# Half-array products of both chunks in one step, waits on GpSimd, more warming products and a new order in a WKV and Fourier-mixing kernel

## The reference

```
for t in range(S):                       # state is 48 x 48 per head
    cur = outer(u * k_t, v_t)
    y_t = r_t @ (state + cur)
    state = w_t[:, None] * state + outer(k_t, v_t)
x = heads side by side                   # 4 x 768 x 384
mixed = real(fft(fft(x, axis=1), axis=2))
u = x + mixed
un = (u - mean(u)) / sqrt(var(u) + 1e-6) # over the last axis
out = u + relu(un @ w_ch1) @ w_ch2
```

## Time and profile before

| | |
|---|---|
| three runs, us | 194.07, 197.35, 198.51 (median 197.35) |
| the profiled execution, us | 195.99, of which its span 194.2 |
| PE, DVE, ACT, POOL busy | 95%, 82%, 64%, 56% |
| HBM read and written | 23.59 MB, 4.72 MB |

### The profile page before, as it was taken

One profiled execution on the slowest core, in us unless ns is written; L12 is line 12 of the kernel. 1 busy time (PEld: TensorE's weight loads), 2 busy tenths in 40 slices (PEclk: granted clock), 3 DMA queues, 4 the chain that ended last, 5 costly groups with the idle time before them and its releaser, 6 DMA issues.

```text
span 194.2 us, 4751 instructions
## 1 busy us (share of the span) xinstructions
PE 184.4 (95%) x1830; PEld 118.5 (61%) x1830; DVE 159.9 (82%) x369; ACT 125.0 (64%) x293; POOL 108.1 (56%) x126
## 2 busy tenths in 40 slices
PE   7997899999997999979999999999899999999994
PEld 3565567577665666656666666765365676656663
DVE  7799985756999798999999999998998889574044
ACT  5799858347997669979778888962682251435200
POOL 2083993646968488486999499446957431000000
PEclk9999969969999999999999999999999999999999
DMA  5998989898998059999859798998475020521133
GB/s 140 312 290 201 217 168 211 152 196 171 177 187 150 0 119 212 204 208 219 185 112 225 124 218 179 192 215 148 91 160 135 0 84 6 130 66 44 41 122 122
DMA packets 107175, 29.79 MB, mean 153 GB/s; under 512 B 102033, under 2 KB 106770, under 8 KB 107154
## 3 DMA queue, kind: packets, MB, share of 16 engines
q1 hardware_dynamic: 105202, 27.14, 64.7%
q0 software_dynamic: 1952, 2.36, 7.5%
HBM read 23.59 MB, written 4.72 MB: 146 GB/s over the span
## 4 chain that ended last, share of the span: by engine, by line
PE 56%; DVE 21%; DMA 11%; issue 3%; ACT 3%; SPq 2%; POOL 2%; DVEq 0%; POOLq 0%
PE bank L1167 16%; PE bank L1149 15%; DMA w<-in_moe_w_ch_dram 6%; PE bank L1188 3%; PE bank L1101 3%; PE bank L1078 3%; DVE ah L817 3%; DMA unt<-un 3%; DMA in_r<-in_r_dram 2%; DVE ah L975 2%; PE bank L1018 2%; DVE x L868 2%; DVE uf L1103 1%; DVE bst L1107 1%; DVE rkh L517 1%
## 5 line engine op out<-in xcount | busy, mean ns | idle before, releaser
L1167 PE MATMUL bank<-w,ht 128*128 128x384 bf16 (+2 forms) x300 | 53.4, 320 | 1.3 <-DMA w<-in_moe_w_ch_dram 1.3
L1149 PE MATMUL bank<-unt,w 128*128 128x384 bf16 x288 | 53.3, 326 | 1.3 <-DVE uf L1103 0.6
L1156 ACT ACTIVATE ht<-bank 128x384 bf16<-128x384 f32 x73 | 33.7, 493 | 20.0 <-PE bank L1149 20.0
L1167 PEld LDWEIGHTS bank<-w,ht 128*128 128x128 bf16 x300 | 27.8, 98 | 17.0 <-DVE ah L817 1.4
L1149 PEld LDWEIGHTS bank<-unt,w 128*128 128x128 bf16 x288 | 26.3, 97 | 18.9 <-DVE uf L1103 1.0
L517 POOL TENSOR_TENSOR rk<-rk,ub 128x384 f32<-128x384 f32 x22 | 22.3, 1019 | 8.7 <-DVE rk L517 4.6
L817 DVE TENSOR_TENSOR ah<-bank,msk 128x512 bf16<-128x512 f32 x36 | 23.3, 678 | 0.9 <-PE bank L812 0.8
L517 POOL TENSOR_TENSOR rkh<-in_k,e 128x384 bf16<-128x384 f32 x14 | 15.7, 1127 | 11.4 <-DMA in_k<-in_k_dram 4.1
L1171 DVE SCALAR_TENSOR_TENSOR osb<-bank,rstd,uf 128x384 f32<-128x384 f32 (+2 forms) x25 | 14.8, 594 | 7.7 <-PE bank L1167 7.6
L517 POOL TENSOR_TENSOR vtd<-in_v,dc 128x384 f32<-128x384 f32 (+1 forms) x21 | 17.4, 830 | 5.5 <-DVE dc L924 3.2
L517 POOL TENSOR_TENSOR rk<-in_r,in_k 128x384 f32<-128x384 f32 x17 | 17.6, 1039 | 1.8 <-issue 1.8
(11 more groups left out here) (167 smaller groups left out, 380.6 us busy)
## 6 DMA issues: line engine op xcount, KB each, us to landing
out_dram<-osb SPq DMA_DIRECT2D x23, 192.0 KB, 2.2
in_v<-in_v_dram SPq DMA_DIRECT2D x18, 192.0 KB, 4.0
in_w<-in_w_dram SPq DMA_DIRECT2D x18, 192.0 KB, 4.1
in_k<-in_k_dram SPq DMA_DIRECT2D x18, 192.0 KB, 4.4
in_r<-in_r_dram SPq DMA_DIRECT2D x18, 192.0 KB, 4.0
w<-in_moe_w_ch_dram POOLq DMA_DIRECT2D x2, 1152.0 KB, 11.0
in_r<-in_r_dram SPq DMA_DIRECT2D x3, 384.0 KB, 5.2
in_w<-in_w_dram SPq DMA_DIRECT2D x3, 384.0 KB, 5.1
```

The costliest lines, as they stand in the source:

```text
L1149: ins = e.matmul(ps(t)[:, 0:384], W1[:, m, 128 * j:128 * j + 128], unt[:, :, m, :], start=(m == 0), stop=(m == NM - 1))
L1156: "act": lambda e, j=j, t=t, ht=ht: e.activation(ht[:, j, :], ps(t)[:, 0:384], ACTF.Relu, scale=-1.0)},
L1167: ins = e.matmul(ps(t)[:, 0:hi - lo], ht[:, j, 128 * x:128 * x + 128], W2[:, j, lo:hi], start=(j == 0), stop=(j == NJ - 1))
```

## The change

1. `tot`, `state` and `ymat` of a pair are each one step for both chunks: the products of chunk 0 (rows 0 to 63) and chunk 1 (rows 64 to 127) alternate, into different PSUM banks. The last pair has no totals and no state for its second chunk.
2. The state-carrying products leave these steps: `inter` (4 full-array products of 96 columns) and the identity product are steps of their own, after the half-array ones. Each of the five chunks after the first has one `inter`, four have an identity product.
3. A POOL step marked `port` waits for the DVE step marked `port` that the plan started last before it (`AHEAD`).
4. Warming products 8 -> 16.
5. Planned durations are changed, and `ORDER` is new for all engines. Counted by step, 124 steps change their engine: 34 from POOL to DVE, 26 from DVE to POOL, 30 from DVE to ACT, 28 from ACT to DVE, 4 from POOL to ACT, 2 from ACT to POOL. POOL has 112 steps instead of 122, 110 of them marked `port`.

Places in the new order that are spoken of below: of batch 0's `xf` folds, six go from POOL to DVE and two from DVE to POOL; its first two `hcr` steps go from POOL to ACT; chunk 5's copy of x from DVE to ACT. W2's DMA has 35 POOL steps ahead of it instead of 39, and the step just ahead but one is now `rkh` of batch 1's chunk 2, whose decay totals stand at PE place 107 (before: 62). On SP the first store of a result stands 43rd (before: 41st), and the load of v for batch 1's chunk 5 stands ahead of it (before: behind it); v of batch 0's last pair is the 21st issue instead of the 15th. Of the 16 warming products, one stands before the first decay sums, four among the first two pairs, six between the second `ymat` and the first product of the mix, five among the first L1101.

```diff
-DMA_T, DMA_U, T_RK, T_UN, T_XFER, T_PAIR, T_SC, T_Y = 15, 2, 1750, 2000, 1800, 1400, 450, 850
+DMA_T, DMA_U, T_RK, T_UN, T_XFER, T_PAIR = 15, 2, 1750, 2000, 1800, 1210
+T_SC, T_Y, T_ST, T_TOT = 250, 1050, 450, 450
...
-NW = 8
+NW = 16
...
+                    if self.AHEAD and e == "pool" and ahead is not None:
+                        s = max(s, ahead.end + self.LAT[e])
...
             if o.port:
                 port[e] = s + o.dur
+                if self.AHEAD and e == "pool" and ahead is not None:
+                    o.deps.add(ahead)
...
+            if o.port and e == "dve":
+                ahead = o
...
-        return int(50 + n * 2.36)
+        return int(50 + n * 2.45)
...
+        nl = 2 - (c0 + 2 == NC)
+        def tot(e):
+            for j in range(nl):
+                e.matmul(ps(tci[j])[:, DM:DM + H], IDB[:, :], NPB[:, :, :].rearrange("p h x -> p (h x)"), start=True,
+                         stop=False, skip_group_check=True)
+            for h in range(HP):
+                for i in range(2):
+                    for j in range(nl):
+                        x = e.matmul(ps(tci[j])[:, DM + 2 * h:DM + 2 * h + 2],
+                                     LB[i2[i]][64 * j:64 * j + 64, 2 * h:2 * h + 2, :].rearrange("t h d -> t (h d)"),
+                                     NON[64 * j:64 * j + 64, :], start=False, stop=(i == 1), skip_group_check=True)
+            return x
+        op("pe", T_TOT, tot, r=["NON", "IDB", "NPB"] + lb, w=tci[0:nl])
...
+        tds = [g.tile("a") for y in range(nl)]
+        def state(e):
+            for h in range(HP):
+                for i in range(2):
+                    for y in range(nl):
+                        x = e.matmul(ps(tds[y])[:, 96 * h:96 * h + 96],
...
+        op("pe", T_ST, state, r=[("KH", i) for i in i4] + vbs, w=tds, tiled=True)
+        ty = [g.tile("a") for y in range(2)]
+        def ymat(e):
+            for i in range(2):
+                for y in range(2):
+                    e.matmul(ps(ty[y])[:, 0:DM], PM[64 * y:64 * y + 64, 4 + i, :], vtb[i][64 * y:64 * y + 64, :],
+                             start=(i == 0), stop=False, skip_group_check=True)
+            for h in range(H):
+                for i in range(2):
+                    for y in range(2):
+                        x = e.matmul(ps(ty[y])[:, D * h:D * h + D], AH[i2[i]][64 * y:64 * y + 64, h, :],
...
+        op("pe", T_Y, ymat, r=ahs + vbs + [("PM", 4), ("PM", 5)] + [("VTD", m % 4) for m in ns], w=ty, tiled=True)
...
+            if c:
+                def inter(e, y=y, s_in=s_in):
+                    for q in range(HP):
+                        x = e.matmul(ps(ty[y])[:, 96 * q:96 * q + 96], RTB[i4[y]][:, q, :], s_in[:, q, :], start=False,
+                                     stop=True, skip_group_check=True)
+                    return x
+                op("pe", mm(96, 4), inter, r=rts + [("ST", (c + 1) % 2)], w=[ty[y]])
+            if y < nl:
+                if c:
+                    op("pe", mm(DM), lambda e, y=y, s_in=s_in: e.matmul(
+                        ps(tds[y])[:, 0:DM], IDB[:, :], s_in[:, :, :].rearrange("p h d -> p (h d)"), start=False, stop=True,
+                        skip_group_check=True), r=[("ST", (c + 1) % 2), "IDB"], w=[tds[y]])
```

More of the change, by code:

```diff
@@ L136 @@
     SWITCH = 95
+    AHEAD = 1
     def __init__(self, nc):
@@ L184, in schedule @@
         port = {"dve": 0, "pool": 0}
+        ahead = None
         bank = [None] * 8
@@ L771, in attention @@
            r=[("RK", i2)], w=[("DC", i2)])
-        op(None, {"pool": 787, "dve": v_1(DM)}, tt(vtd[:, :, :], vt[:, :, :],
+        op(None, {"pool": 820, "dve": v_1(DM)}, tt(vtd[:, :, :], vt[:, :, :],
                                                    dc[:, :].unsqueeze(2).to_broadcast([128, H, D]), ALU.mult),
@@ L898, in attention_pair @@
             op("act", a_ps(DM) + 20, lambda e, t=tce[j]: e.activation(ps(t)[:, 0:DM], ps(t)[:, 0:DM], ACTF.Exp), w=[tce[j]])
-        for j in range(2):
-            last = c0 + j == NC - 1
-            if not last:
-                def tot(e, j=j, t=tci[j]):
-                    e.matmul(ps(t)[:, DM:DM + H], IDB[:, :], NPB[:, :, :].rearrange("p h x -> p (h x)"), start=True,
-                             stop=False, skip_group_check=True)
-                    for h in range(HP):
-                        for i in range(2):
-                            x = e.matmul(ps(t)[:, DM + 2 * h:DM + 2 * h + 2],
-                                         LB[i2[i]][64 * j:64 * j + 64, 2 * h:2 * h + 2, :].rearrange("t h d -> t (h d)"),
-                                         NON[64 * j:64 * j + 64, :], start=False, stop=(i == 1), skip_group_check=True)
-                    return x
-                op("pe", mm(1, 9), tot, r=["NON", "IDB", "NPB"] + lb, w=[tci[j]])
-            ne = DM if last else DM + H
+        nl = 2 - (c0 + 2 == NC)
[11 more added lines that the diff above has]
+        op("pe", T_TOT, tot, r=["NON", "IDB", "NPB"] + lb, w=tci[0:nl])
+        for j in range(2):
+            ne = DM + H if j < nl else DM
             op("act", a_ps(ne), lambda e, j=j, ne=ne, t=tci[j]: e.activation(E2[i2[j]][:, 0:ne], ps(t)[:, 0:ne], ACTF.Exp,
@@ L926, in attention_pair @@
                r=[("RK", z)], w=[("DC", z)])
-            op(None, {"pool": 787, "dve": v_1(DM)}, tt(vtb[j].rearrange("p (h d) -> p h d", d=D), cut("v", j),
+            op(None, {"pool": 820, "dve": v_1(DM)}, tt(vtb[j].rearrange("p (h d) -> p h d", d=D), cut("v", j),
                                                        dc[:, :].unsqueeze(2).to_broadcast([128, H, D]), ALU.mult),
@@ L980, in attention_pair @@
         vbs = [("VB", n % 4) for n in ns]
+        tds = [g.tile("a") for y in range(nl)]
[4 more added lines that the diff above has]
+                        x = e.matmul(ps(tds[y])[:, 96 * h:96 * h + 96],
+                                     KH[i4[i]].rearrange("t h d -> t (h d)")[64 * y:64 * y + 64, 128 * h:128 * h + 128],
+                                     VB[ns[i] % 4][64 * y:64 * y + 64, 2 * h:2 * h + 2, :].rearrange("t h d -> t (h d)"),
+                                     start=(h == 0 and i == 0), stop=(i == 1), skip_group_check=True)
+            return x
@@ new lines, in attention_pair @@
+        op("pe", T_ST, state, r=[("KH", i) for i in i4] + vbs, w=tds, tiled=True)
[9 more added lines that the diff above has]
+                        x = e.matmul(ps(ty[y])[:, D * h:D * h + D], AH[i2[i]][64 * y:64 * y + 64, h, :],
+                                     VB[ns[i] % 4][64 * y:64 * y + 64, h, :], start=False, stop=(i == 1),
+                                     skip_group_check=True)
+            return x
@@ L981, in attention_pair @@
+        op("pe", T_Y, ymat, r=ahs + vbs + [("PM", 4), ("PM", 5)] + [("VTD", m % 4) for m in ns], w=ty, tiled=True)
         for y in range(2):
-            c, n = c0 + y, ns[y]
-            p0, p1 = 64 * y, 64 * y + 64
+            c = c0 + y
             s_in, s_out = ST[(c + 1) % 2], ST[c % 2]
-            ty = g.tile("a")
-            if c < NC - 1:
-                tds = g.tile("a")
-                def state(e, c=c, p0=p0, p1=p1, s_in=s_in, tds=tds):
-                    if c:
-                        e.matmul(ps(tds)[:, 0:DM], IDB[:, :], s_in[:, :, :].rearrange("p h d -> p (h d)"),
-                                 start=True, stop=False, skip_group_check=True)
-                    for h in range(HP):
-                        for i in range(2):
-                            x = e.matmul(ps(tds)[:, 96 * h:96 * h + 96],
-                                         KH[i4[i]].rearrange("t h d -> t (h d)")[p0:p1, 128 * h:128 * h + 128],
-                                         VB[ns[i] % 4][p0:p1, 2 * h:2 * h + 2, :].rearrange("t h d -> t (h d)"),
-                                         start=(c == 0 and i == 0), stop=(i == 1), skip_group_check=True)
-                    return x
-                op("pe", mm(96, 8) + (mm(DM) if c else 0), state, r=[("KH", i) for i in i4] + vbs
-                   + ([("ST", (c + 1) % 2), "IDB"] if c else []), w=[tds])
-                op("dve", v_1(DM), lambda e, y=y, tds=tds, s_out=s_out: e.tensor_tensor(
@@ new lines, in attention_pair @@
+            if c:
[3 more added lines that the diff above has]
+                                     stop=True, skip_group_check=True)
+                    return x
+                op("pe", mm(96, 4), inter, r=rts + [("ST", (c + 1) % 2)], w=[ty[y]])
[4 more added lines that the diff above has]
+                        skip_group_check=True), r=[("ST", (c + 1) % 2), "IDB"], w=[tds[y]])
+                op("dve", v_1(DM), lambda e, y=y, s_out=s_out: e.tensor_tensor(
@@ L1003, in attention_pair @@
                     out=s_out[:, :, :].rearrange("p q x -> p (q x)").rearrange("p (h d) -> p h d", d=D),
-                    in0=ps(tds)[:, 0:DM].rearrange("p (h d) -> p h d", d=D),
+                    in0=ps(tds[y])[:, 0:DM].rearrange("p (h d) -> p h d", d=D),
```

(19 more changed lines are left out.)

## The result

The changed kernel takes 185.57 us (median of 4 runs, 184.34 to 187.21) where the kernel before takes 196.17 beside it (4 runs, 194.07 to 198.51). The profiled execution of after took 187.21 us (span 185.4, clock 0.982).

The account below looks back on a forecast made before the run. PE was taken as the bound, with batch 0's recurrence waiting for it. 6.6 us saved on PE became 5 into the mix, some 4 past W2, plus 1 for SP's load: 196.0 - 5.0 = 191.0 us, range 187.0 to 197.5.

Parts of the forecast that it names:

- the waits: POOL steps waiting for DVE steps: at most some 5 us gain on DVE, loss possible; taken as 0.
- the order: SP's load of v going ahead of a result store: 1 us (0 to 2); other engine changes nearly cancel before batch 0's mix.
- the clock's: PE's two early clock dips: about one stays away, gain 1.0 us, ends +3.4 and -3.4.
- `ymat`, `state`, `tot`: PE steps before batch 0's mix, joined per pair: gains of 5.6, 0.7 and 0.3 us.
- The 0.1 us per meeting: In the old `ymat`, 0.8 us lost where half-array and full-array products meet, eight times, 0.1 each.
- I carry 5 us into the mix: Before batch 0's mix: 6.6 us saved on PE, 6.0 that DVE can give back, 5 us counted.
- Warming, -1.0: Eight more warming products on PE: cost between 0 and 1.3 us, taken as 1.0.
- some 4 of the 5 us pass the gate: W2's transfer, issued at 45 to 46 us, lands 3.5 to 4.5 us sooner, passing some 4 us on.
- The gain didn't end at W2: Rival: W2 lands hardly earlier, PE waits 5 us more; 195 to 196 us; chance 0.27 together with the clock.
- The halves do overlap: Rival: half-array products in PE's new steps don't overlap; about 193 us; chance 0.1.
- cold stretch: Rival: PE waits for DVE, loses its clock twice more, 3.4 us back; 194 to 195; chance 0.27 together with W2.
- the slower case: Rival: POOL's waits delay PE from 70 to 140 us; 199 to 204 us; chance 0.12; sign: waits above 16 us.

Follow-up runs that it names:

- e14: Changed kernel with four unused whole-array products put between the narrow ones of each of the three output steps: 183.40 and 185.32 us at clock 1.0, ratio 0.955.
- e3: Kernel before with only the new forms of the PE steps; old order, no waits, 8 warming products: 191.22 us, ratio 0.990.
- e12: Old order with the new step forms and no waits, plus one SyncE load moved ahead of the first result store: 189.74 us, ratio 0.985.
- e13: Changed kernel with the load of v for batch 1's chunk 5 put back behind the first result store: 184.85 us, ratio 0.957.
- e5: Changed kernel without any of the 16 warming products: 183.68 and 184.23 us at clock 1.0, ratio 0.959.
- e11: Changed kernel without alternating the halves and without the 16 warming products: 184.41 us, ratio 0.946.
- a3: Changed kernel run again with no edit, as reference in the fourth sitting: 181.97 and 185.94 us at clock 1.0, 186.19 at .991, 191.45 at .982.
- a2: Changed kernel run again with no edit, in the second sitting: 184.45 us, ratio 0.960.
- e4: Changed kernel with the old forms of the PE steps; new order, waits and 16 warming products kept: 199.86 us, ratio 1.026.
- e6: Changed kernel without alternation: each chunk's products in turn in totals, state and output steps: 183.17 us, ratio 0.952.
- e1: Changed kernel without POOL's waits on DVE; plan, order and steps kept: 186.29 us, ratio 0.966.

## Why the prediction was wrong

The direction was right, the time was not: 191.0 was forecast, with 187.0 as the lowest of the range, and 185.57 was measured. Two terms failed, the waits, which were put at 0, and the order, put at 1.0 us; the clock's was too small. Step by step:

- **`ymat`, `state`, `tot`: right on PE.** 0.83 against 1.0 us, 0.53 and less against 0.5, 0.47 against 0.6. Three output steps and five `inter` at some 0.2 make 3.5 us where 4.4 was forecast and 10.0 stood before: 6.5 saved, inside the ends of 3.5 and 6.7. The 0.1 us per meeting was right (e14). The forecast took the Trainium skill's overhead of some 60 cycles a product ("TensorEngine Tiling (Array Packing)", "Instruction Overhead") to mean that alternating 48 columns brings nothing; 0.0153 against 0.0256 us apart shows that it does, on PE. The products of one half still stand 0.031 apart (2 x 0.0153) when they alternate, so the rows don't speak against the Trainium skill, only against that reading.
- **"I carry 5 us into the mix": too high for the forms alone.** In e3 the first product with `hcs` came 3.8 us sooner (line below; before 45.6) and that execution ended 5.0 sooner (191.04 us at .991, before 195.99 at .982), of which a part is the second dip of the clock, gone in e3; at a clock of 1.0 the forms gave 2.5 and by the ratio 2.0 [0.2, 3.8]. DVE, which before had waited for PE, became the bound: PE sits idle for 2.2 of e3's 30.7 us, having been busy for 30.52 of them before, and on the chain that ended last, from 9 us to that product, e3 has 17.0 us of DVE and 9.9 of PE, before 11.8 and 21.6.

```profile
41.79 1.14 PE L1117 MATMUL bank<-dtm,hcs 128*128 128x384 bf16 x6
```

- **"The waits on POOL ... I take 0": failed.** They give 1.2 to 2.5 us by the ratios, 1.9 to 3.2 at an equal clock. The step had the right mean (0.700) and the right bound ("at most some 5 us on DVE"; measured 4.3), and then argued that a wait only settles who goes first. It does, and that is the gain: blocked, a DVE step takes 1.40 instead of 0.56 us, and DVE is full where POOL has time. The mean of 0.700 hid that: before, the median `rkh` took 0.553 and the longest 1.12. The 0.549 set beside it is not a step with two SBUF operands, as the text has it, but `st`, which reads a PSUM bank; the median gives the same number.
- **The order: failed.** It was priced at 1 us, for the one load; that load gives some 0.3 to 0.5 between the mixes (e12, e13), and the order as a whole 3.3 to 4.6 by the ratios, 2.9 at clock 1.0. "Engine changes of the rest nearly cancel there", said the forecast of those of the 124 moves that lie ahead of the first mix; it did not ask which engine binds once PE is shorter, and so what a new division of work between DVE, ACT and POOL is worth.
- **The clock, +1.0 with ends of 3.4: right in sign.** Before ran at 1.0 in two of its 29 runs, in 191.64 and 191.78 us, some 4 us below its median of 195.5; the changed kernel's median, 185.1, is 0.7 above its time at 1.0. So the clock is worth some 3 us between the kernels as they usually run, inside the ends and more than the 1.0 taken. Why the old forms let it fall is open: the meetings added in e14 alone don't.
- **Warming, -1.0: too high.** Nothing shows at a full clock (e5, e11).
- **W2.** Issued at 41.3, not 45 to 46; first user at 54.9, not 58. That "some 4 of the 5 us pass the gate" was right in kind: 8.1 us sooner at the issue, 7.0 at the user.
- **The rivals.** The gain didn't end at W2. The halves do overlap. One cold stretch of 6.8 us came at W2's wait in the profiled execution, another of 6.8 in a3's, behind a wait of 4.7 us for ACT, none in a2. POOL's waits for DVE between 70 and 140 us did pass the 16 us named as the sign of the slower case (17.0 in the seven largest rows of after, two of which follow), and PE was busy for 70.00 of these 70 us all the same. So that sign was badly chosen: POOL waited in time that it had.

```profile
POOL rk L527 <- DVE rk L527: 6.2, 2, 4.9
POOL xf L527 <- DVE xf L527: 2.6, 1, 2.6
```

In the sum at clock 1.0: the 4 us carried past W2 for forms, warming and clock became 2.5 for the forms; 0 became 1.9 for the waits; 1 became 2.9 for the order. These make 7.3, and with some 3 us of clock the 10 that lie between the medians. The range ended past PE's best case and had neither DVE's 5 us, named in its own text, nor more than 2 us of the order in it.

## What to carry to other kernels

When a step is made shorter, price the new bound before the saving: the steps' 6.5 us on PE were worth 2 to 2.5 at an equal clock, put in alone, and what took load off DVE next was worth more. Take parts out of the finished kernel as well as putting them into the old one: the same forms were worth 12.9 us there, because the rest does not pay without them. A mean above the usual duration on one of two engines that share a path should be opened into its single instructions: a few that are blocked whole are a term of the sum, and a wait on the engine with time to spare takes them away. A list of moves in an order is not priced by the one move that is easy to see.

## What the runs showed of the hardware

- PE stood at 1.2 GHz for 30.7 us while its products covered 29.04 of them (e4): a busy share near one does not say that the clock is up.
- Half-array products that alternate between the halves overlap: four of 384 columns take 0.34 us to the next start, where two of one half and the meeting behind them took 0.43 before; those of 48 columns stand 0.0153 us apart, and 0.0256 when one half is used in a row (e6).
- A meeting of half-array and whole-array products costs 0.10 us on PE (e14).
- In the case shown, a VectorE step with two SBUF operands that starts 0.02 us behind GpSimd's takes 1.40 us instead of 0.56 (e1, after).
- Some 2.7 us of added PE work among the recurrence steps, in three places, left the first product with `hcs` where it was, 38.25 us beside 38.22 and 38.62 (e14, a2, a3).
